# Attention and two expert stages on one core: a mask and some casts put elsewhere in the order, and the first gates spread by TensorE

## The reference, cut to what matters

```
# q, k, v: 4 x 8 heads x 576 x 64, f: 4 x 8 x 576 gates
cum = cumsum(log(clip(f, 1e-4, 1)))                      # along the sequence
scores = q @ k.T / 8 + cum[i] - cum[j], masked above the diagonal
attn = softmax(scores); x = attn @ v                     # 2304 tokens x 512
h = x @ w_in; g = piecewise(h); y = g @ w_out            # 512 -> 2048 -> 512
logits = normalize(y) @ normalize(expert_emb).T / tau    # 8 experts
out = gate * (relu(y @ w1[e]) @ w2[e]) for the chosen expert e of each token
```

## Time and profile before

| what | value |
|---|---|
| time, median of 3 runs | 849.34 us (848.88 to 849.74) |
| the profiled execution's own time | 848.67 us |
| its span, first to last instruction | 846.5 us |
| mean granted TensorE clock | 0.996 |
| busy: PE, PEld, DVE, ACT, POOL | 98%, 92%, 49%, 46%, 42% |
| attention, about | 0 to 204 us |

### The profile page before, as it was taken

One profiled execution on the slowest core, in us unless ns is written; L12 is line 12 of the kernel. 1 busy time (PEld: TensorE's weight loads), 2 busy tenths in 40 slices (PEclk: granted clock), 3 DMA queues, 4 the chain that ended last, 5 costly groups with the idle time before them and its releaser, 6 DMA issues.

```text
span 846.5 us, 13803 instructions
## 1 busy us (share of the span) xinstructions
PE 831.4 (98%) x5018; PEld 778.9 (92%) x5019; DVE 410.8 (49%) x1002; ACT 392.9 (46%) x916; POOL 353.0 (42%) x366
## 2 busy tenths in 40 slices
PE   7999999999999999999999999999999999999996
PEld 5888888889999999999999999999998998998985
DVE  5888888887555454454444444455534110110200
ACT  6777877876665444534544534433332121111121
POOL 5776778856665020211111202074311692010295
PEclk9999999999999999999999999999999999999999
DMA  7577988962000310301211033252222354304041
GB/s 223 189 246 232 288 264 285 291 207 57 29 1 2 102 57 29 104 29 56 75 56 57 1 103 106 75 163 63 76 101 87 120 167 125 87 37 125 26 138 42
DMA packets 70941, 95.62 MB, mean 113 GB/s; under 512 B 7174, under 2 KB 47110, under 8 KB 70864
## 3 DMA queue, kind: packets, MB, share of 16 engines
q1 hardware_dynamic: 62688, 80.33, 31.3%
q10 hardware_dynamic: 6416, 9.59, 3.2%
q0 software_dynamic: 1760, 4.72, 1.5%
HBM read 70.87 MB, written 24.27 MB: 112 GB/s over the span
## 4 chain that ended last, share of the span: by engine, by line
PE 96%; DVE 2%; DMA 1%; issue 1%; ACT 0%; POOL 0%; POOLq 0%; DVEq 0%; SPq 0%; ACTq 0%
PE psum L1523 25%; PE psum L1525 24%; PE psum L1524 24%; PE psum L1494 6%; PE psum L1450 5%; PE psum L1477 5%; PE psum L1455 2%; PE psum L1447 1%; PE psum L1431 1%; DVE pr L1112 1%; PE psum L1606 1%; PE psum L1590 0%; PE psum L1591 0%; DMA c<-cum_d 0%; DVE ptl L1134 0%
## 5 line engine op out<-in xcount | busy, mean ns | idle before, releaser
L1523 PE MATMUL psum<-xh,winh 128*128 128x384 f32 x384 | 129.0, 336 | 0.0
L1523 PE MATMUL psum<-gh,wouth 128*128 128x384 f32 x384 | 128.3, 334 | 0.2 <-issue 0.2
L1525 PE MATMUL psum<-xh,winl 128*128 128x384 f32 x384 | 128.4, 334 | 0.0
L1524 PE MATMUL psum<-xl,winh 128*128 128x384 f32 x384 | 128.3, 334 | 0.0
L1525 PE MATMUL psum<-gh,woutl 128*128 128x384 f32 x384 | 128.3, 334 | 0.0
L1524 PE MATMUL psum<-gl,wouth 128*128 128x384 f32 x384 | 128.3, 334 | 0.0
L898 ACT ACTIVATE hpos<-psum,minus 128x384 f32<-128x384 f32 x96 | 55.9, 582 | 142.3 <-DVE hclip L1160 142.1
L1165 DVE TENSOR_TENSOR g<-hpos,hsq 128x384 f32<-128x384 f32 x96 | 64.5, 672 | 109.2 <-ACT hsq L900 109.2
L691 POOL TENSOR_TENSOR xst<-xst 128x384 f32<-128x384 f32 x24 | 24.7, 1031 | 178.4 <-DMA xst<-rinv_d 178.2
L1270 DVE SCALAR_TENSOR_TENSOR hl<-psum,hh 128x384 fp32r<-128x384 f32 x48 | 26.8, 558 | 139.4 <-ACT hh L954 139.4
L1169 DVE TENSOR_TENSOR gl<-g,gh 128x384 fp32r<-128x384 f32 x96 | 64.1, 668 | 61.0 <-ACT gh L931 61.0
(11 more groups left out here) (233 smaller groups left out, 1871.6 us busy)
## 6 DMA issues: line engine op xcount, KB each, us to landing
praw<-moe_w SPq DMA_DIRECT2D x48, 256.0 KB, 2.8
qraw<-q SPq DMA_DIRECT2D x15, 448.0 KB, 4.5
vraw<-vk SPq DMA_DIRECT2D x16, 320.0 KB, 3.8
xh<-yh_d SPq DMA_DIRECT2D x20, 256.0 KB, 4.2
xl<-yl_d SPq DMA_DIRECT2D x20, 256.0 KB, 4.6
kraw<-k SPq DMA_DIRECT2D x16, 288.0 KB, 3.8
xa_d<-xo SPq DMA_DIRECT2D x16, 288.0 KB, 4.0
xb_d<-xo SPq DMA_DIRECT2D x16, 288.0 KB, 4.5
```

Of the source, the lines that this page charges most:

```text
L1523: nc.tensor.matmul(psum_at, ah, bh, start=start, stop=False)
L1524: nc.tensor.matmul(psum_at, ah, bl, start=False, stop=False)
L1525: return nc.tensor.matmul(psum_at, al, bh, start=False, stop=stop)
```

## The change

Block 1's mask is issued behind block 2's products (MASK_LATER), and its minimum is taken a step later on VectorE. ScalarE's casts go ahead of the exponential in the steps of blocks 5, 7 and 8. Block 0's low part goes one step later on VectorE. The gates of pair 0 no longer go over HBM: TensorE multiplies two rows of `fc` with a 2 x 128 matrix of ones and zeros (`spread`, built by GpSimd), and ScalarE copies the result to `c8`. The normalization of the embeddings, their transposes and copies move three or four steps later.

```
-    CASTS_FIRST = 5
+    CASTS_FIRST = (5, 7, 8)
...
+        spread = rturn[0:2, 0, :]
...
-                for h in range(2 if p else 1):
+                for h in range(2):
...
             sp.dma_start(cum_d, fc).then_inc(cum_out, 16)
-            sp.wait_ge(cum_out, 16)
-            load_c(0)
             load_k(1)
             load_v(0)
...
             load_first(1)
+            sp.wait_ge(cum_out, 16)
             load_c(1)
...
+            nc.gpsimd.memset(spread, 1.0).then_inc(spread_ok, 1)
+            pool.wait_ge(spread_ok, 1)
+            nc.gpsimd.affine_select(out=spread, in_=spread, compare_op=ALU.is_ge, fill=0.0, base=0,
+                                    pattern=[[1, P]], channel_multiplier=-D).then_inc(spread_ok, 1)
+            pool.wait_ge(spread_ok, 2)
+            nc.gpsimd.affine_select(out=spread, in_=spread, compare_op=ALU.is_ge, fill=0.0, base=D - 1,
+                                    pattern=[[-1, P]], channel_multiplier=D).then_inc(spread_ok, 1)
             pool.wait_ge(cum_out, 16)
+            pool.wait_ge(c_spread, 1)
...
-            act.wait_ge(cum_out, 16)
-            act.dma_start(c8[D:P, 0, :], cum_d[1:2, :].to_broadcast([D, S])).then_inc(c_in[0], 16)
+            act.wait_ge(c_spread, 1)
+            nc.scalar.copy(c8[:, 0, :].rearrange("p (a c) -> p a c", a=2), psum[:, PX:PY + 1, 0:S // 2]).then_inc(c_first, 1)
...
-                if i != CASTS_FIRST and 0 <= n + 2 < STEPS:
+                if i not in CASTS_FIRST and 0 <= n + 2 < STEPS:
                     exp(n + 2)
...
-                if i == CASTS_FIRST and 0 <= n + 2 < STEPS:
+                if i in CASTS_FIRST and 0 <= n + 2 < STEPS:
                     exp(n + 2)
...
-                if n == 1:
+                if n == 4:
                     act.wait_ge(en_turned, 1)
...
-                if i == 0:
-                    dve.wait_ge(c_in[p % 2], 32 * (p // 2 + 1))
+                if n == 0:
+                    dve.wait_ge(c_first, 1)
+                elif i == 0:
+                    dve.wait_ge(c_in[p % 2], 32 * ((p + 1) // 2))
...
-                m = tile_of(n + 3)[1]
-                if m != 1 and 0 <= n + 3 < STEPS:
+                if 0 <= n + 3 < STEPS:
                     masked(n + 3)
-                if m == 0 and 0 <= n + 4 < STEPS:
-                    masked(n + 4)
...
-                    for k in fills_of(i):
+
+                    for k in fills_of(i) if i not in (1, 2) else fills_of(i - 1):
                         low(p, k)
...
-                if n == -AHEAD:
+                if n == 0:
                     step(nc.vector.reciprocal(tau_inv[:], tau_sb[:]))
...
-                if n == 2:
+                if n == 5:
                     dve.wait_ge(ent_h, 1)
...
+            pe.wait_ge(cum_ok, 1)
+            pe.wait_ge(spread_ok, 3)
+            for j in range(2):
+                x = nc.tensor.matmul(psum[:, PX + j, 0:S // 2], spread, fc[0:2, j * (S // 2):(j + 1) * (S // 2)],
+                                     start=True, stop=True)
+            x.then_inc(c_spread, 1)
...
-            MASK_LATER = (4,)
+            MASK_LATER = (1, 4)
...
-                if n == 0:
+                if n == 3:
                     pe.wait_ge(en_ok, 1)
```

More of the change, by code:

```diff
@@ L269, in attention_moe_kernel @@
         f_in = sem("f_in"); clip_ok = sem("clip_ok"); log_ok = sem("log_ok"); cum_ok = sem("cum_ok")
+        spread_ok = sem("spread_ok"); c_spread = sem("c_spread"); c_first = sem("c_first")
         cum_done = sem("cum_done"); cum_out = sem("cum_out")
```

## The result

The changed kernel takes 841.35 us in the median of four runs (840.63 to 842.12); the kernel before, on the same chip, 849.54 (848.88 to 850.49). The ratio is 0.9903, 95% interval 0.9886 to 0.992. I had forecast 841.1 with a range of 838.3 to 845.2. The profiled execution took 841.62 us, with a span of 839.5: 7.05 us less than the profiled one of before. The sum was right; of its terms only that of the casts was, and the errors of the others cancelled, which is luck.

What follows compares the result with a forecast made beforehand. TensorE holds 96% of the chain of waits, so the span is its work plus holes. Gains 1.5 + 3.9 + 0.35 + 3.1 - 0.6 = 8.25 us off 848.67 give 840.4, plus 0.67 for the median 841.1 us; range 838.3 to 845.2.

Steps and rivals of the forecast that it cites:

- Casts ahead: ScalarE's casts before exponentials at blocks 7 and 8: closes the hole ahead of block 4's scores, 13 x 0.30 = 3.9 us.
- Block 8's wait: Block 0's low part one step later on VectorE, so block 8's scores no longer wait for block 6's minimum: 3.1 us.
- some 0.3 us are left: Margin of block 6's minimum before TensorE asks for it, in the eight pairs splitting x; nothing left in the slowest.
- a meeting now and then: VectorE meeting a GpSimd instruction in later pairs; with later loads, 0.6 us taken off the gain.
- Block 1's mask: Block 1's mask behind block 2's products, its minimum a step later: taken as 0 us, upper bound 1.3.
- Opening: First gates spread by TensorE instead of over memory, normalization moved: gain 1.5 us, bounds 0 and 2.3.
- the clock would hold: At the opening, no half clock expected at 14 to 16 us; sign: granted clock 1.0 from 12 to 18 us.
- opening gains nothing: Rival: in the opening, moved normalization and table load take the place of the DMA; 842.6 us, chance 0.12.
- The second pair: Denominators' sum held by GpSimd makes a 0.74 us hole; may miss or meet it, half counted, 0.35 us.
- The allowance of 0.6: Deduction of 0.6 us in later pairs, for loads with less room and for a meeting now and then.
- Port, once: Rival: denominators' sum waits for a GpSimd instruction; 848.2 us in all pairs, chance 0.04, or 843.8 in four, 0.07.
- Loads: Rival: the eight pairs loading x can't be shorter than 11.56 us, 3.7 come back; 844.8 us, chance 0.09.

Runs made afterwards that it cites:

- (2): The changed kernel with ScalarE's casts ahead of the exponential in block 5's step alone, not at blocks 7 and 8: 845.57 us, ratio 0.996 to the kernel before.
- (3): The changed kernel with casts ahead of the exponential at blocks 5 and 7, not at block 8: 844.99 us, ratio 0.9947 to the kernel before.
- (4): The changed kernel with block 0's low part in its own step again, ahead of block 6's minimum: 843.34 us, ratio 0.993 to the kernel before.
- (1): The changed kernel with block 1's mask right behind its own product again, its minimum still a step later: 841.93 us, ratio 0.9913 to the kernel before.
- (5): The kernel before with the later pairs' edits alone (mask, casts, low part, block 1's minimum) and the old opening: 841.48 us, ratio 0.9906 to the kernel before.
- (8): The changed kernel with 14 instead of 22 products on constants at the start: 839.23 us, ratio 0.9887 to the kernel before.
- (7): The changed kernel without the addition of 1e-9 to the row sums, the inverse reading the sums: 841.01 us, ratio 0.9904 to the kernel before.
- (6): The changed kernel with VectorE's share of the x split two steps later: 842.26 us, ratio 0.9915 to the kernel before.
- number 9: The changed kernel once more, with no edit: 841.00 us, ratio 0.9899 to the kernel before.
- number 10: The changed kernel with 14 products on constants, and square root, table load and embeddings' normalization ahead of the first minimum: 838.51 us, ratio 0.9871 to the kernel before.

## Why the prediction was right

- **Casts ahead.** Right in mechanism and size: 13 x 0.30 in the profile. Undone with the other edits in place (2) they cost 5.5 in holes and 4.2 in time, so the edits are not independent: what the moved mask brings at the sixth fill is lost there again as long as the casts are late. That block 8's edit keeps the late heads fed is shown by (3), and was stated without a price.
- **Block 8's wait.** Mechanism right (4), size too large: 3.1 forecast, 1.5 in the profile. The step that failed is the remainder for "a meeting now and then" and "some 0.3 us are left". I took 0.94 to 1.12 for a split that meets GpSimd from where it stood before, 7.28 us into a pair, beside a cast of q of 0.94. The change brings it to 6.84 us, beside the split of k of 1.43, and it takes up to 1.63. Of the eight pairs three wait, by 0.34 to 0.75.
- **Block 1's mask.** I took 0 and kept 1.3 as the bound above; the measured value is 1.0 to 1.2, by the traces and not by the times (1). I set the mask's own 0.03 against the second one's 0.03 and looked at the start of the next group, not at the whole way from product to heads, which is 0.26 with a mask in between and 0.15 without.
- **Opening.** 1.5 forecast, 0.55 in the profile, and in time nothing (5). Two sizes were off. The two products take 1.16 and not 1.0, and they start when the constants' products end, at 9.71 to 10.68 in the eight profiles and not at 9.28. The 9.28 was misread: in the trace of before it is the start of the last product on constants, these end at 9.66, and the first scores start at 9.49. From there on the steps came as written: copy 0.64, table load right behind, normalization 1.6 us between block 3's and 4's minima. That the clock would hold came true, but it brought nothing that shows: the kernel with the half clock (5) takes the same time. Two of the signs that I had named failed: the first minimum came at 12.08 and not near 11.2, and block 4's at 15.03, later than the 14.9 that I had put down as a sign of being wrong. The rival "opening gains nothing" named the table load and the normalization; by these runs it was the start, since fewer products on constants bring pair 1's first scores 1.6 us forward (8).
- **The second pair.** The meeting stayed (1.40 us, the hole 0.87), and my half of 0.74 with it. Without the sum the hole goes (7).
- **The allowance of 0.6** was for loads and for a meeting now and then. No later pair is lengthened by loads (11.01 and its wait at block 8 make up each); the meetings cost 1.8 us, three times the allowance, and are counted under block 8.
- **Rivals.** "Port, once" did not happen to the denominators' sum in the changed kernel's later pairs beyond 0.54 us; (6) shows it is real. Of its kind was what happened to the split of x. "Loads" is out: pairs with x reach 11.01, one of them (85.66 to 96.67) at a DMA share of 0.91. The Trainium skill (SBUF — State Buffer, "SBUF: two separate sides") counts VectorE operations with two SBUF inputs among those that contend, against a GpSimd operation that reads SBUF. The splits of 1.60 and 1.96 us above, which have two such inputs, agree with a wait for the whole of the other's instruction: both end 0.4 us after it. The sum of 1.42 us ends 0.03 after it, but has one SBUF input, which is not the case of that sentence. That the one that starts first wins is not borne out by the profiled starts. In the earlier trace rows VectorE's split ran though it came 0.20 us second, in number 9 it ran 0.04 us behind GpSimd's split of k (0.54 us, at 104.37), and in number 10 it waited when 0.19 behind (1.66 us, at 100.75). What decides it stays open.

The total of 8.25 forecast against 8.19 in the medians is luck: opening, block 8, second pair and mask were off by -0.95, -1.6, -0.5 and +1.2, the allowance, its meetings booked under block 8, gave +0.6, and 1.1 lies between the gain of the profiled executions (7.05) and that of the medians, within the interval.

## What to carry to other kernels

Where one engine is busy all the time, compare the same stretch in the first period and in a later one, start to start: holes of 0.2 to 0.4 us stand in no list of waits, and thirteen of them were half of this gain. When a hole is closed, work out what the next piece of work waits for, with the period already shortened; of two edits the first brought 0.6 us and both together 4.2, because the first only moved the wait 2 us on. VectorE's split of x had the price of whatever it met at GpSimd, so when the place of such an instruction moves, look up who is running there, and put nothing urgent behind it.

## What I had not expected of the hardware

Profiles differ at the very start, where nothing was changed: the 22 products on constants took 6.68 to 7.76 us in ten of them (7.23 and 7.42 in the two of the changed kernel). Their starts are first 0.43 us apart and then 0.22, at a granted clock of 1.00 in the rows of both stretches, and what differs is how many come at the slower pace: in the changed kernel's profile the first eleven distances, in the ten profiles 8 to 13. With the gates' products behind them this shift of up to 1 us goes into the start of pair 1.

An instruction of 0.54 us on VectorE took up to 1.96 us beside GpSimd, 1.4 us more.
